# Scores at distances of 4 and 16 tokens: whole request rows in plain runs of columns instead of interleaved blocks with four columns in each skipped

## The chip, the cores and the metric

The kernel runs on one core of one Trainium2 chip, in one launch. The metric is the device time of the whole launch in microseconds (us); lower is better. Engines are named as in the profile: PE is TensorE (PEld its weight loads), DVE is VectorE, ACT is ScalarE, POOL is GpSimd, SP is SyncE, which here only issues DMAs.

## The reference

The program is a gated linear attention followed by two feed-forward layers:

```python
# q, k, v, alpha: batch 4, heads 8, sequence 768, head dim 48
for t in range(S):
    state = alpha[:, :, t, :, None] * state + einsum('bhd,bhe->bhde', k[:, :, t], v[:, :, t])
    y[:, :, t] = einsum('bhd,bhde->bhe', q[:, :, t], state)
x = y as (3072 tokens, 384)
h = x @ w_in;  x = (h * sigmoid(1.702 * h)) @ w_out       # 384 -> 2048 -> 384
h = x @ w_in2; out = (h - tanh(h)) @ w_out2               # 384 -> 2048 -> 384
```

All inputs and outputs are fp32.

## The kernel before

**Attention in chunks.** The sequence of a head is cut into 12 chunks of 64 tokens. Two batches with their eight heads (16 sequences, in 8 slots of two heads each) form a unit for one chunk; there are 24 units, each worked on as two items of half the slots, 48 items in all. Within a chunk the output of a token is a sum over earlier tokens of the same chunk, weighted by scores, and a part from the state of the chunk before. A score between two tokens needs the product of all alphas between them, so the kernel builds scores by levels: pairs that differ in the last base-4 digit of the token number (level 1), in the middle digit (level 4) and in the first digit (level 16). At each level the request rows (queries times alpha products) are made for digit distances 1, 2 and 3, and multiplied on PE with keys that carry the products on their side. The 64 tokens of a chunk lie in memory in the order `ORDER`, digits reversed.

**Request rows.** `R1`, `R4` and `R16` hold, for each slot, the columns for the three levels. Level 1 has plain runs of columns. `R4` has 112 columns a slot as four blocks of 28: 16 columns for distance 1, 8 for distance 2 and 4 for distance 3. `R16` has 112 columns as sixteen blocks of 7: 4, 2 and 1. A token whose digit is below the distance has no partner at it, so of the distance-1 columns of a block the first quarter is never used as a score. These columns exist all the same because the next products start from them. The views of these tiles are made in `views` (L368 to L388). The products are made by DVE for unit 0 in `first_unit` (L1082, product helper at L1087) and by POOL for the others in `first_part` and `second_part` (L519 and L548, product helper at L512). ACT copies the plain queries into the first 16 columns (L831).

**Scores on PE.** For an item PE runs `scores_1` (L618, 160 columns), the state products (L631), and then `scores_4_16` (L636): the matmuls at L645 take from `R4` the 24 used columns of each of the four blocks, those at L655 from `R16` the 6 used columns of each of the sixteen, so 96 moving columns in both. There are 8 matmuls of each line in an item, in two rounds of four. The four of a round go to four different quarters of the array (two halves of rows by two halves of columns, `TILES`). Each fp32 matmul shows in the trace as two instructions, so each line has 16 in an item and 768 in all. The results lie in PSUM as 96 columns for level 4 and 96 for level 16, block by block as in the request rows.

**Scores on DVE.** `scores` (L1034) builds the 64x64 score matrix of an item: one masked product for the diagonal (L1038), then nine predicated copies (L1056), three distances for each of the three levels, each with a mask of its own from the tile `MASK`. They are in a strict order (`put_step`); the fourth waits for `z_done`, which PE raises after `scores_4_16`. Destination, mask and PSUM source are all cut into blocks: 1 block at level 1, 4 at level 4, 16 at level 16.

**Order of the work.** The first two items (`LEAD`) are computed before any feed-forward product. All others are visits: `visits` (L128) gives each a place in the stream of feed-forward products on PE (L736, L741 up, L765 down; from the third token block on each fp32 product is three fp32r products). At a visit PE first finishes the item before (`item_outputs`: key transposes L604, state part L691, values L700), after waiting for its scores, then starts the next (`item_scores`). The stream is in program order, so all that PE does in a visit comes ahead of the next feed-forward product. The visits end near half of the span; after that PE runs feed-forward products only. Before the first feed-forward product SP sends the outputs of the first two items to HBM, loads them back as the first token block (`load_x`, L441), and behind that issues loads of alpha, queries, keys and the next weight groups (L317, L330) from one queue.

Of the kernel before, what the change touches and what calls it, by code (L numbers as in the profile page):

```python
# [37 lines left out]
PX = HS + D  # L38


def head_rows(hd):
    return slice(hd * HS, hd * HS + D)


C = 64
# [10 lines left out]
R1W = 64 + 32 + 16 + 64  # L56
S1W = R1W - 16
RW = 64 + 32 + 16
NW = 48 + 32 + 16
SLOT = 16  # L60

QP = 4
SL = 2 * QP
# [17 lines left out]
def level_masks():  # L81

    token = np.array(ORDER)
    j = np.tile(token, 2)[:, None]
    cols = []
    for h in (1, 4, 16):
        run = 4 * {1: 16, 4: 4, 16: 1}[h]
        for block in token.reshape(C // run, run):
            for dist in (1, 2, 3):
                cols.append(j // h == block[None, dist * run // 4:] // h - dist)  # L90
        if h == 1:
            cols.append(j == token[None, :])
    return np.concatenate(cols, axis=1).astype(np.int32)


MASK_AT = {1: 0, 4: S1W, 16: S1W + NW}
MASKW = S1W + 2 * NW


def item_of(j):  # L100
# [77 lines left out]
def build(nc, qT, kT, aT, vL, w_in1, w_out1, w_in2, w_out2, masks, ident, head, outT):  # L178
# [3 lines left out]
    with ctx:  # L182
# [27 lines left out]
        R4 = [sb(f"r4_{u}", [PX, SL, RW], where=att) for u in U2]  # L210
        R16 = [sb(f"r16_{u}", [PX, SL, RW], where=att) for u in U2]
# [12 lines left out]
        F4 = sb("f4", [PX, SL, 8, 4], where=att)  # L224
# [4 lines left out]
        MASK = sb("mask", [P, MASKW], I32, where=att)  # L229
# [7 lines left out]
        pZ = [pb(f"pZ{n}", [P, 4, 256]) for n in U2]  # L237
        pS1 = [x[:, :, 0:S1W] for x in pX]
        pP = [x[0:PX, :, S1W:S1W + D] for x in pX]
        pS4 = [z[:, :, 0:NW] for z in pZ]  # L240
        pS16 = [z[:, :, NW:2 * NW] for z in pZ]
        pY = [z[0:PX, :, 0:C] for z in pZ]
        pKT = [z[:, :, C:C + D] for z in pZ]
        pKT0 = [x[:, :, S1W + D:S1W + 2 * D] for x in pX]
# [5 lines left out]
        def buf(j):  # L250

            return int(j == 1)
# [30 lines left out]
        block = ctx.enter_context(nc.Block())  # L283
# [84 lines left out]
        def views(U):  # L368

            r1, r4, r16, q64 = R1[U % 2], R4[U % 2], R16[U % 2], Q64[U % 2]  # L370
            by4, by16 = (x[:].rearrange("p c (a x) -> p c a x", a=a) for x, a in ((r4, 4), (r16, 16)))
            r16 = r16[:]
            return Views(
                al=AL[:].rearrange("p (c s b) -> p c s b", c=SL, s=4),
                slot=r1[:, :, 0:7 * SLOT].rearrange("p c (k b) -> p c k b", b=SLOT),
                q=r1[:, :, R1W - C:R1W].rearrange("p c (s b) -> p c s b", s=4),
                qd4=by4[:, :, :, 0:16],
                v4=by4[:, :, :, 0:16],
                d4=by4[:, :, :, 16:24],
                e4=by4[:, :, :, 24:28],  # L380
                t4=T4[:].rearrange("p c s b -> p c (s b)"),
                pf4=F4[:, :, None, 0:4, :].to_broadcast([PX, SL, 4, 4, 4]),
                q16=r16.rearrange("p c (a b x) -> p c a b x", a=4, b=4)[:, :, :, :, 0:4],
                v16=by16[:, :, :, 0:4],
                d16=by16[:, :, :, 4:6],
                e16=by16[:, :, :, 6],
                pf16=F16[:, :, None, 0:4].to_broadcast([PX, SL, 16, 4]),
                q64=q64[:].rearrange("p (c a x) -> p c a x", c=SL, x=4))  # L388

# [120 lines left out]
        def _(pool):  # L510
            def mul(out, in0, in1):
                nc.gpsimd.tensor_tensor(out, in0, in1, ALU.mult).then_inc(q_step, 1)  # L512
# [35 lines left out]
            def second_part(U):  # L548
                base, tbase = U * Q_STEPS, U * T_STEPS
                r = views(U)  # L550
                pool.wait_ge(q_step, base + 5)
                pool.wait_ge(q4_copied, U + 1)
                pool.wait_ge(t_step, tbase + T_PF4)
                mul(r.q16, r.v4.rearrange("p c a (b x) -> p c a b x", b=4), r.pf4)
                mul(r.d4, r.v4[:, :, :, 8:16], r.t4[:, :, None, 4:12].to_broadcast([PX, SL, 4, 8]))
                pool.wait_ge(q_step, base + 6)
                pool.wait_ge(t_step, tbase + T_T16)
                mul(r.d16, r.v16[:, :, :, 2:4], T16[:, :, None, 1:3].to_broadcast([PX, SL, 16, 2]))
                pool.wait_ge(q_step, base + 7)
                mul(r.e4, r.d4[:, :, :, 4:8], r.t4[:, :, None, 4:8].to_broadcast([PX, SL, 4, 4]))  # L560
                pool.wait_ge(q_step, base + 8)
                mul(r.e16, r.d16[:, :, :, 1], T16[:, :, 1:2].to_broadcast([PX, SL, 16]))

                pool.wait_ge(t_step, tbase + T_SF16)
                if U >= 2:
                    pool.wait_ge(y_done, 2 * U - 2)
                nc.gpsimd.tensor_tensor(r.q64, r.v16, r.pf16, ALU.mult).then_inc(q64_ready, 1)
# [25 lines left out]
        def _(pe):  # L593
# [42 lines left out]
            def scores_4_16(j):  # L636
                U, pp = item_of(j)[:2]
                u = U % 2
                if pp == 0:
                    pe.wait_ge(q_step, U * Q_STEPS + Q_R4)  # L640
                    pe.wait_ge(k4_ready, U + 1)
                for q in range(2):
                    for h, z in TILES:
                        s = z * QP + 2 * pp + q
                        last = nc.tensor.matmul(pS4[buf(j)][z * C:(z + 1) * C, 2 * h + q, :].rearrange("p (a x) -> p a x", a=4),  # L645
                                                K4[u][head_rows(h), s * C:(s + 1) * C],
                                                R4[u][head_rows(h), s, :].rearrange("p (a x) -> p a x", a=4)[:, :, 4:],
                                                start=True, stop=True)
                if pp == 0:
                    pe.wait_ge(q_step, U * Q_STEPS + Q_R16)  # L650
                    pe.wait_ge(k16_ready, U + 1)
                for q in range(2):
                    for h, z in TILES:
                        s = z * QP + 2 * pp + q
                        last = nc.tensor.matmul(pS16[buf(j)][z * C:(z + 1) * C, 2 * h + q, :].rearrange("p (a x) -> p a x", a=16),  # L655
                                                K16[u][head_rows(h), s * C:(s + 1) * C],
                                                R16[u][head_rows(h), s, :].rearrange("p (a x) -> p a x", a=16)[:, :, 1:],
                                                start=True, stop=True)
                last.then_inc(z_done, 1)

            def item_scores(j):
# [278 lines left out]
        def _(dve):  # L940
# [93 lines left out]
            def scores(j, beside):  # L1034
                step = j * PUTS
                x = buf(j)
                dve.wait_ge(x_done, j + 1)
                nc.vector.tensor_tensor(AT[x], pS1[x][:, :, S1W - C:S1W],  # L1038
                                        MASK[:, None, S1W - C:S1W].to_broadcast([P, 4, C]), ALU.mult
                                        ).then_inc(put_step, 1)  # L1040
                puts = 0
                for h, ps in ((1, pS1[x]), (4, pS4[x]), (16, pS16[x])):
                    nb = C // (4 * {1: 16, 4: 4, 16: 1}[h])
                    run = C // nb
                    for dist in (1, 2, 3):
                        w = (4 - dist) * run // 4
                        at0 = (0, 3, 5)[dist - 1] * run // 4
                        dst = AT[x].rearrange("p k (b x) -> p k b x", b=nb)[:, :, :, dist * run // 4:run]
                        src = ps[:, :, 0:NW].rearrange("p k (b x) -> p k b x", b=nb)[:, :, :, at0:at0 + w]
                        msk = MASK[:, MASK_AT[h]:MASK_AT[h] + NW].rearrange("p (b x) -> p b x", b=nb)[:, :, at0:at0 + w]  # L1050
                        if h == 4 and dist == 1:
                            beside()
                            dve.wait_ge(z_done, j + 1)
                        puts += 1
                        dve.wait_ge(put_step, step + puts)
                        nc.vector.copy_predicated(dst, msk[:, None, :, :].to_broadcast([P, 4, nb, w]), src)\  # L1056
                            .then_inc(scores_ready if puts == PUTS else put_step, 1)
# [24 lines left out]
            def first_unit():  # L1082

                r = views(0)

                def mul(out, in0, in1):
                    nc.vector.tensor_tensor(out, in0, in1, ALU.mult).then_inc(q_step, 1)  # L1087
# [18 lines left out]
                dve.wait_ge(q_step, 5)  # L1106
                dve.wait_ge(q4_copied, 1)
                dve.wait_ge(t_step, T_T16)
                mul(r.q16, r.v4.rearrange("p c a (b x) -> p c a b x", b=4), r.pf4)
                mul(r.d4, r.v4[:, :, :, 8:16], r.t4[:, :, None, 4:12].to_broadcast([PX, SL, 4, 8]))  # L1110
                dve.wait_ge(q_step, 6)
                mul(r.d16, r.v16[:, :, :, 2:4], T16[:, :, None, 1:3].to_broadcast([PX, SL, 16, 2]))
# [103 lines left out]
```

## Time and profile before

| | |
|---|---|
| median of 3 runs | 978.55 us (978.42 to 978.98) |
| the profiled execution's own time | 978.98 us |
| its span, first to last instruction | 977.2 us |
| mean granted TensorE clock | 0.991 |
| PE busy | 952.2 us (97%) |
| DVE busy | 544.2 us (56%) |
| ACT busy | 334.1 us (34%) |
| POOL busy | 282.5 us (29%) |
| DMA | 59.07 MB, mean 60 GB/s |

The span is shorter than the execution's time by 1.8 us, which lie around the first and the last instruction. Busy time of an engine is time in which at least one of its instructions runs. The granted clock is a share of full speed: 1.00 stands for 2.4 GHz and 0.50 for 1.2 GHz. Durations of single matmuls overlap, since they are pipelined; what counts on PE is how far apart they start.

### The profile page before, as it was taken

The numbers are of one execution on the slowest core, as the hardware profiler recorded it, in microseconds if no ns is written. First come the engines' busy times: TensorE is split into PE (matmuls) and PEld (weight loads), VectorE is DVE, ScalarE is ACT, GpSimd is POOL, SyncE is SP. The second block draws the span as 40 slices with busy tenths as digits, with TensorE's granted clock in tenths as the row PEclk, the third lists the DMA queues.
The fourth block names the chain that finished last, engine by engine and source line by source line (L and its number), as shares of the span: only waits on it lengthen the run. The fifth ranks groups of instructions, "written<-read, shape, count | busy, mean of one in ns | idle before, by whom it ended". The sixth has DMA issues, their size and how long they took to land.

```text
span 977.2 us, 22232 instructions
## 1 busy us (share of the span) xinstructions
PE 952.2 (97%) x9342; PEld 823.7 (84%) x9342; DVE 544.2 (56%) x1349; ACT 334.1 (34%) x683; POOL 282.5 (29%) x314
## 2 busy tenths in 40 slices
PE   4799999999999999999999999999999999999998
PEld 3799999999999988888888888888888888888886
DVE  7679998878888877776321224334334333343333
ACT  2342333332332332323234554333333333333332
POOL 2554656555665655444001542000000000000000
PEclk9699999999999999999999999999999999999999
DMA  7833242332332432321113322020020010200000
GB/s 159 251 76 73 57 101 55 88 76 55 95 75 55 111 65 56 102 46 23 15 62 122 98 81 89 1 65 1 1 66 1 5 60 1 65 1 1 33 1 33
DMA packets 136533, 59.07 MB, mean 60 GB/s; under 512 B 114288, under 2 KB 131824, under 8 KB 136432
## 3 DMA queue, kind: packets, MB, share of 16 engines
q1 hardware_dynamic: 133616, 55.54, 22.6%
q10 hardware_dynamic: 2816, 2.10, 0.7%
q8 instruction: 74, 1.21, 0.5%
q14 instruction: 27, 0.22, 0.1%
HBM read 43.45 MB, written 14.16 MB: 59 GB/s over the span
## 4 chain that ended last, share of the span: by engine, by line
PE 94%; DVE 3%; DMA 1%; SPq 1%; issue 1%; ACT 0%; DVEq 0%; ACTq 0%
PE pX L741 38%; PE pZ L765 27%; PE pX L765 14%; PE pX L618 3%; PE pX L736 2%; PE pZ L700 2%; PE pZ L645 2%; PE pZ L604 2%; PE pZ L655 1%; PE pX L631 1%; PE pZ L691 1%; DVE scores L1056 1%; DMA w_raw<-w_out 1%; DVE w_lo L1062 1%; SPq L317 0%
## 5 line engine op out<-in xcount | busy, mean ns | idle before, releaser
L741 PE MATMUL pX<-x_hi,w_hi 128*128 128x512 f32 (+2 forms) x624 | 227.7, 365 | 0.7 <-ACT g L906 0.7
L741 PE MATMUL pX<-x_lo,w_hi 128*128 128x512 f32 (+2 forms) x624 | 227.3, 364 | 0.0
L741 PE MATMUL pX<-x_hi,w_lo 128*128 128x512 f32 (+2 forms) x624 | 227.3, 364 | 0.0
L1072 DVE TENSOR_TENSOR g_lo<-g,g_hi 128x512 fp32r<-128x512 f32 (+2 forms) x208 | 133.3, 641 | 155.0 <-ACT g_hi L911 154.8
L1171 DVE TENSOR_TENSOR g<-pX,sg 128x512 f32<-128x512 f32 x96 | 66.3, 691 | 177.7 <-ACT sg L908 177.7
L765 PE MATMUL pZ<-g_hi,w_hi 128*128 128x512 f32 (+2 forms) x414 | 151.0, 365 | 0.0
L765 PE MATMUL pZ<-g_lo,w_hi 128*128 128x512 f32 (+2 forms) x414 | 150.8, 364 | 0.0
L765 PE MATMUL pZ<-g_hi,w_lo 128*128 128x512 f32 (+2 forms) x414 | 150.8, 364 | 0.0
L911 ACT ACTIVATE g_hi<-g 128x512 fp32r<-128x512 f32 (+2 forms) x208 | 121.3, 583 | 78.0 <-DVE g L1171 74.5
L906 ACT ACTIVATE g<-pX 128x512 f32<-128x512 f32 (+3 forms) x144 | 65.6, 456 | 210.1 <-PE pX L741 175.9
L741 PEld LDWEIGHTS pX<-x_hi,w_hi 128*128 128x128 f32 x624 | 117.5, 188 | 17.8 <-ACT g L906 1.1
L741 PEld LDWEIGHTS pX<-x_lo,w_hi 128*128 128x128 f32 x624 | 117.5, 188 | 16.9
L741 PEld LDWEIGHTS pX<-x_hi,w_lo 128*128 128x128 f32 x624 | 117.5, 188 | 16.8
L908 ACT ACTIVATE sg<-pX 128x512 f32<-128x512 f32 x96 | 57.4, 598 | 181.9 <-PE pX L741 181.9
L512 POOL TENSOR_TENSOR r<-r,alpha 112x128 f32<-112x128 f32 (+2 forms) x115 | 109.2, 965 | 18.9 <-DMA r<-q_t 15.3
L1056 DVE COPY_PREDICATED scores<-mask,pZ 128x192 f32<-128x192 int32 (+2 forms) x282 | 105.7, 375 | 9.0
L765 PEld LDWEIGHTS pZ<-g_hi,w_hi 128*128 128x128 f32 x414 | 77.9, 188 | 11.3
L765 PEld LDWEIGHTS pZ<-g_lo,w_hi 128*128 128x128 f32 x414 | 78.0, 188 | 11.2
L765 PEld LDWEIGHTS pZ<-g_hi,w_lo 128*128 128x128 f32 x414 | 78.0, 188 | 11.2
L765 PE MATMUL pX<-g_hi,w_hi 128*128 128x512 f32 (+2 forms) x207 | 79.4, 384 | 0.0
L765 PE MATMUL pX<-g_hi,w_lo 128*128 128x512 f32 (+2 forms) x207 | 75.5, 364 | 0.0
L765 PE MATMUL pX<-g_lo,w_hi 128*128 128x512 f32 (+2 forms) x207 | 75.4, 364 | 0.0
(95 smaller groups left out, 1136.9 us busy)
## 6 DMA issues: line engine op xcount, KB each, us to landing
v<-v_l SPq DMA_DIRECT2D x96, 48.0 KB, 2.6
x_raw<-hidden SPq DMA_DIRECT2D x6, 768.0 KB, 5.8
attn_out<-y SPq DMA_DIRECT2D x94, 48.0 KB, 1.8
out_t<-o SPq DMA_DIRECT2D x10, 384.0 KB, 3.4
alpha<-a_t SPq DMA_DIRECT2D x24, 128.0 KB, 3.0
r<-q_t SPq DMA_DIRECT2D x24, 128.0 KB, 3.0
k<-k_t SPq DMA_DIRECT2D x24, 128.0 KB, 3.0
w_raw<-w_in SPq DMA_DIRECT2D x16, 192.0 KB, 2.4
```

The lines of the kernel that those rows point to most:

```text
L512: nc.gpsimd.tensor_tensor(out, in0, in1, ALU.mult).then_inc(q_step, 1)
L604: last = nc.tensor.matmul(out[z * C:(z + 1) * C, 2 * (h ^ z) + q, :], K64[U % 2][head_rows(h), s * C:(s + 1) * C], IDN[head_rows(h), :], s ...
L618: last = nc.tensor.matmul(pS1[buf(j)][z * C:(z + 1) * C, 2 * h + q, :], K1[u][head_rows(h), s * C:(s + 1) * C], R1[u][head_rows(h), s, SLO ...
L645: last = nc.tensor.matmul(pS4[buf(j)][z * C:(z + 1) * C, 2 * h + q, :].rearrange("p (a x) -> p a x", a=4), K4[u][head_rows(h), s * C:(s + ...
L741: last = nc.tensor.matmul(pH(N)[:, 0:w], win(wp, f, m), XS[T % 2][xp][:, m, 0:w], start=(n == 0), stop=(n == len(terms) - 1))
L765: last = nc.tensor.matmul(pO[m][:, 0:w], wt[:, m * P:(m + 1) * P], g, start=(f == 0 and n == 0), stop=(f == NF - 1 and n == len(terms) - 1))
L906: nc.scalar.activation(g_raw(N), H0[:, 0:width(T)], ACT.Gelu_apprx_sigmoid).then_inc(g_done, 1)
L908: nc.scalar.activation(SG[N % 2][:], pH(N), ACT.Tanh).then_inc(sg_done, 1)
L911: nc.scalar.activation(GH[:, columns(N)], g_raw(N), ACT.Copy).then_inc(gh_done, 1)
L1056: nc.vector.copy_predicated(dst, msk[:, None, :, :].to_broadcast([P, 4, nb, w]), src)\
L1072: nc.vector.tensor_tensor(GL[:, columns(N)], g_raw(N), GH[:, columns(N)].bitcast(F32), ALU.subtract).then_inc(gl_done, 1)
L1171: nc.vector.tensor_tensor(g_raw(N), pH(N), SG[N % 2][:], ALU.subtract).then_inc(g_done, 1)
```

## The change

The columns of `R4` and `R16` are laid out by distance: 64 columns for distance 1, 32 for distance 2, 16 for distance 3, each run in token order. Both matmuls read the whole 112 columns of a slot in one run and write 112 columns to PSUM, 16 of them (the distance-1 columns of tokens with digit 0) never read afterwards. The predicated copies of levels 4 and 16 skip these by a step (`skip`) at distance 1, and read mask and PSUM in a plain run at distances 2 and 3. Their destination, the number of elements and their count stay as they are. The masks grow by 2 x 16 columns. Level 1 is unchanged.

```diff
-NW = 48 + 32 + 16
@@ level_masks
+    digit = {1: np.arange(C) // 16, 4: np.arange(C) // 4 % 4, 16: np.arange(C) % 4}
     for h in (1, 4, 16):
-        run = 4 * {1: 16, 4: 4, 16: 1}[h]
-        for block in token.reshape(C // run, run):
-            for dist in (1, 2, 3):
-                cols.append(j // h == block[None, dist * run // 4:] // h - dist)
+        for dist in (1, 2, 3):
+            least = dist if h == 1 or dist > 1 else 0
+            i = token[digit[h] >= least][None, :]
+            cols.append(j // h == i // h - dist)
-MASK_AT = {1: 0, 4: S1W, 16: S1W + NW}
-MASKW = S1W + 2 * NW
+MASK_AT = {1: 0, 4: S1W, 16: S1W + RW}
+MASKW = S1W + 2 * RW
@@ PSUM views
-        pS4 = [z[:, :, 0:NW] for z in pZ]
-        pS16 = [z[:, :, NW:2 * NW] for z in pZ]
+        pS4 = [z[:, :, 0:RW] for z in pZ]
+        pS16 = [z[:, :, RW:2 * RW] for z in pZ]
@@ views
-                qd4=by4[:, :, :, 0:16],
-                v4=by4[:, :, :, 0:16],
-                d4=by4[:, :, :, 16:24],
-                e4=by4[:, :, :, 24:28],
+                qd4=r4[:, :, 0:C].rearrange("p c (s b) -> p c s b", s=4),
+                v4=r4[:, :, 0:C].rearrange("p c (a x) -> p c a x", a=4),
+                d4=r4[:, :, C:C + 32].rearrange("p c (a x) -> p c a x", a=4),
+                e4=r4[:, :, C + 32:RW].rearrange("p c (a x) -> p c a x", a=4),
-                q16=r16.rearrange("p c (a b x) -> p c a b x", a=4, b=4)[:, :, :, :, 0:4],
-                v16=by16[:, :, :, 0:4],
-                d16=by16[:, :, :, 4:6],
-                e16=by16[:, :, :, 6],
+                q16=r16[:, :, 0:C].rearrange("p c (a x) -> p c a x", a=4),
+                v16=r16[:, :, 0:C].rearrange("p c (a x) -> p c a x", x=4),
+                d16=r16[:, :, C:C + 32].rearrange("p c (a x) -> p c a x", x=2),
+                e16=r16[:, :, C + 32:RW],
@@ second_part (POOL) and first_unit (DVE)
-                mul(r.q16, r.v4.rearrange("p c a (b x) -> p c a b x", b=4), r.pf4)
+                mul(r.q16, r.v4, r.pf4)
@@ scores_4_16
-                        last = nc.tensor.matmul(pS4[buf(j)][z * C:(z + 1) * C, 2 * h + q, :].rearrange("p (a x) -> p a x", a=4),
+                        last = nc.tensor.matmul(pS4[buf(j)][z * C:(z + 1) * C, 2 * h + q, :],
-                                                R4[u][head_rows(h), s, :].rearrange("p (a x) -> p a x", a=4)[:, :, 4:],
-                                                start=True, stop=True)
+                                                R4[u][head_rows(h), s, :], start=True, stop=True)
...
-                                                R16[u][head_rows(h), s, :].rearrange("p (a x) -> p a x", a=16)[:, :, 1:],
-                                                start=True, stop=True)
+                                                R16[u][head_rows(h), s, :], start=True, stop=True)
@@ scores
-                        at0 = (0, 3, 5)[dist - 1] * run // 4
+                        if h == 1:
+                            at0, wide, skip = (0, 48, 80)[dist - 1], w, 0
+                        else:
+                            at0 = (0, C, C + 32)[dist - 1]
+                            wide, skip = (run, run // 4) if dist == 1 else (w, 0)
-                        src = ps[:, :, 0:NW].rearrange("p k (b x) -> p k b x", b=nb)[:, :, :, at0:at0 + w]
-                        msk = MASK[:, MASK_AT[h]:MASK_AT[h] + NW].rearrange("p (b x) -> p b x", b=nb)[:, :, at0:at0 + w]
+                        src = ps[:, :, at0:at0 + nb * wide].rearrange("p k (b x) -> p k b x", b=nb)[:, :, :, skip:wide]
+                        msk = MASK[:, MASK_AT[h] + at0:MASK_AT[h] + at0 + nb * wide]
+                        msk = msk.rearrange("p (b x) -> p b x", b=nb)[:, :, skip:wide]
```

## Rows read from the trace of the kernel before

**Rows 1.** The page: the chain that ended last, share of the span by engine.
```profile
PE 94%; DVE 3%; DMA 1%; SPq 1%; issue 1%; ACT 0%; DVEq 0%; ACTq 0%
```

**Rows 2.** Waits of PE: engine line <- releaser: us in total, times, longest us.
```profile
PE pX L736 <- ACT g L906: 5.0, 3, 4.2
...
PE pZ L604 <- DVE scores L1056: 0.6, 1, 0.6
```

**Rows 3.** PE by stretches: from:to length, busy (instructions), granted clock, DMA share, GB/s.
```profile
36.64:46.00 9.36, 8.63 (x119) 0.50 0.92 302
...
46.00:104.50 58.50, 58.50 (x1052) 1.00 0.39 87
104.50:114.00 9.50, 8.80 (x165) 1.00 0.23 43
114.00:353.00 239.00, 239.00 (x3920) 1.00 0.34 76
```

**Rows 4.** Single lines: instructions, duration ns min/median/max, first and last start, form.
```profile
L618 PE MATMUL pX<-r,k x768: 294/296/525, 7.9 to 472.7; 48*64 48x160 f32 x192
...
L691 PE MATMUL pZ<-q,state x704: 216/216/311, 42.7 to 482.3; 48*48 48x64 f32 x176
...
L645 PEld LDWEIGHTS pZ<-r,k x768: 129/133/228, 11.4 to 473.2; 48*64 48x64 f32 x192
L645 PE MATMUL pZ<-r,k x768: 242/243/419, 11.4 to 473.2; 48*64 48x96 f32 x192
...
L655 PE MATMUL pZ<-r,k x768: 242/242/365, 12.1 to 473.6; 48*64 48x96 f32 x192
```

**Rows 5.** The chain in one visit: start us, us that it advances, what.
```profile
60.69 0.23 PE pZ L691 x16
...
62.71 0.33 PE pZ L655 x16
```

**Rows 6.** The chain in the scores of the first two items, same columns.
```profile
13.10 0.38 DVE scores L1056
...
16.85 0.38 DVE o L1056
...
17.26 0.31 DVE o L1056
...
17.59 0.24 DVE o L1056
...
17.85 0.45 DVE o L1056
...
18.32 0.45 DVE o L1056
...
18.80 0.44 DVE o L1056
```

**Rows 7.** Timeline around first score products: start, us, engine, line, out<-in, count.
```profile
11.09 0.28 DVE L1087 TENSOR_TENSOR r<-r,t 112x128 f32<-112x128 f32 x1
...
11.29 0.38 DVE L1087 TENSOR_TENSOR r<-r,t 112x128 f32<-112x128 f32 x1
...
12.12 0.86 PE L655 MATMUL pZ<-r,k 48*64 48x96 f32 x16
```

**Rows 8.** The chain behind the first two items, same columns.
```profile
23.51 0.41 SPq L317
...
28.18 7.69 DMA w_raw<-w_out
```

**Rows 9.** The chain from 99 us to 114 us, start us, us, what.
```profile
100.73 0.34 DVE scores L1038
...
109.89 0.35 DVE scores L1038
...
113.96 0.45 PE pZ L604 x16
```

**Rows 10.** Waits of POOL, as in group 2.
```profile
POOL k L527 <- DVE g_lo L1072: 100.3, 18, 7.8
```

More of the change, by code:

```diff
@@ L370, in views @@
             r1, r4, r16, q64 = R1[U % 2], R4[U % 2], R16[U % 2], Q64[U % 2]
-            by4, by16 = (x[:].rearrange("p c (a x) -> p c a x", a=a) for x, a in ((r4, 4), (r16, 16)))
-            r16 = r16[:]
             return Views(
@@ L376, in views @@
                 q=r1[:, :, R1W - C:R1W].rearrange("p c (s b) -> p c s b", s=4),
-                qd4=by4[:, :, :, 0:16],
-                v4=by4[:, :, :, 0:16],
-                d4=by4[:, :, :, 16:24],
-                e4=by4[:, :, :, 24:28],
+                qd4=r4[:, :, 0:C].rearrange("p c (s b) -> p c s b", s=4),
+                v4=r4[:, :, 0:C].rearrange("p c (a x) -> p c a x", a=4),
+                d4=r4[:, :, C:C + 32].rearrange("p c (a x) -> p c a x", a=4),
+                e4=r4[:, :, C + 32:RW].rearrange("p c (a x) -> p c a x", a=4),
                 t4=T4[:].rearrange("p c s b -> p c (s b)"),
-                pf4=F4[:, :, None, 0:4, :].to_broadcast([PX, SL, 4, 4, 4]),
-                q16=r16.rearrange("p c (a b x) -> p c a b x", a=4, b=4)[:, :, :, :, 0:4],
-                v16=by16[:, :, :, 0:4],
-                d16=by16[:, :, :, 4:6],
-                e16=by16[:, :, :, 6],
+                pf4=F4[:, :, 0:4, :].rearrange("p c s b -> p c (s b)")[:, :, None, :].to_broadcast([PX, SL, 4, 16]),
+                q16=r16[:, :, 0:C].rearrange("p c (a x) -> p c a x", a=4),
+                v16=r16[:, :, 0:C].rearrange("p c (a x) -> p c a x", x=4),
+                d16=r16[:, :, C:C + 32].rearrange("p c (a x) -> p c a x", x=2),
+                e16=r16[:, :, C + 32:RW],
                 pf16=F16[:, :, None, 0:4].to_broadcast([PX, SL, 16, 4]),
@@ L654, in scores_4_16 @@
                         s = z * QP + 2 * pp + q
-                        last = nc.tensor.matmul(pS16[buf(j)][z * C:(z + 1) * C, 2 * h + q, :].rearrange("p (a x) -> p a x", a=16),
+                        last = nc.tensor.matmul(pS16[buf(j)][z * C:(z + 1) * C, 2 * h + q, :],
                                                 K16[u][head_rows(h), s * C:(s + 1) * C],
-                                                R16[u][head_rows(h), s, :].rearrange("p (a x) -> p a x", a=16)[:, :, 1:],
-                                                start=True, stop=True)
+                                                R16[u][head_rows(h), s, :], start=True, stop=True)
                 last.then_inc(z_done, 1)
@@ L1108, in first_unit @@
                 dve.wait_ge(t_step, T_T16)
-                mul(r.q16, r.v4.rearrange("p c a (b x) -> p c a b x", b=4), r.pf4)
+                mul(r.q16, r.v4, r.pf4)
                 mul(r.d4, r.v4[:, :, :, 8:16], r.t4[:, :, None, 4:12].to_broadcast([PX, SL, 4, 8]))
```

## The prediction

> **What bounds the kernel now.** I read the page's busy times and chain first. PE is busy for 97% of the span (the table above) and makes up 94% of the chain that ended last, against 3% for DVE [rows 1]. So I read the PE side in two views: who PE waits for, and how full it is by stretches. From 46.0 to 104.5 us and from 114 to 353 us PE has no idle time [rows 3]. Between them lie 0.70 idle us [rows 3], of which 0.6 are one wait for a DVE score copy [rows 2], ahead of the visit at 113.96. Ahead of 46 us the order of things is another one: the chain runs through DVE's work for the first two items [rows 6], then through SP's queue and a weight load that lands 7.69 us after its issue [rows 8], and PE waits 4.2 us for what comes of it [rows 2]. The reader is to see three regimes: a head that DVE's products and copies set, a weight load whose start they set, and from about 36 us a PE stream in which every added nanosecond of PE counts.
>
> **Part 1, wider matmuls (adds, on the path).** L645 and L655 go from 96 to 112 moving columns. A column's price: the 160-column instruction takes 296 ns, the 96-column one 243 [rows 4], 53 ns for 64 columns, 0.83 ns a column, so 13.2 ns for 16. The four quarters of the array work beside each other, so the price is paid once for four instructions, four times for the 16 of a line. The chain agrees: L655 advances it by 0.33 us for its 16, L691 with 64 columns by 0.23 [rows 5], 0.10 us for 32 columns, 0.05 for 16. I take 4 x 13.2 = 53 ns a line, 0.106 us a visit. PE's program order puts it ahead of the next feed-forward product, and nothing of PE's idle time hides it.
> Of 48 items, items 0 and 1 lie in the head, and item 2 (at 29 us) ends before the 4.2 us wait, so it costs nothing. Item 3 runs at about 45 us at granted clock 0.50, the 1.2 GHz level [rows 3], where a column costs double: 0.2 us. The other 44 run at 1.00: 44 x 0.106 = 4.65 us. Sum +4.85 us.
> The unknown is whether the old reads in pieces (24 of 28, or 6 of 7 columns) cost something that a plain run doesn't. Two lines with plain runs stand on both sides: L691 with 64 columns takes 216 ns, L618 with 160 takes 296 [rows 4]. The straight line between them gives 242.7 ns at 96 columns, and L645 and L655 have 243 and 242. So the pieces cost nothing, whether of 24 or of 6, and 112 columns will take 256. Ends: the chain's 0.10 us is read to 0.01, so 0.045 to 0.058 us a line, or +4.1 to +5.3 in the sum; for a gain the pieces would have to cost what the straight line excludes (rival B).
>
> **Part 2, DVE's predicated copies (less time).** In item 1 the three copies of level 4 took 0.38, 0.31 and 0.24 us, for 192, 128 and 64 elements a partition. Those of level 16, with the same numbers of elements, took 0.45, 0.45 and 0.44 [rows 6]. The time of level 16 doesn't follow the elements: it has 64 pieces of 3, 2 and 1. After the change mask and source are plain runs at distances 2 and 3, and the destination stays in pieces. From both sides: nothing if the destination sets the price; 0.07 + 0.14 + 0.20 = 0.41 us an item if all three fall to level 4's times. The nearest row for one side of it: the product of 128 elements that is written and read in steps of 7 took 0.38 us, the one in pieces of four 0.28 [rows 7], 0.8 ns an element. So I put distance 2 at 0.33 and distance 3 at 0.27 and leave distance 1 at 0.45, where all three streams keep their pieces. That is 0.29, I take 0.3 us an item. Level 4 stays: its pieces cost nothing now.
> The Trainium skill (SBUF — State Buffer, section "Door 1: The DMA port swizzle", the note on cachelines) says that SBUF is read in lines of 16 bytes and PSUM in lines of 8, and that each step to a new line costs. The trace agrees in kind for DVE, as far as 0.44 against 0.24 us for 64 elements shows it. By it the stepping destination would keep a price, which lies between my ends.
> Where does the saving count? In the steady stretch DVE has half its time free, so nowhere, but for two places.
> *Head.* The chain runs through both items' copies. The product in steps of 7 (L1087 at 11.29) gives back 0.1 us, but the fourth copy of item 0 starts at 13.10, and PE's L655 ends at 12.12 + 0.86 = 12.98 [rows 6, 7]. So the fourth copy waits for PE already. PE there is slower: L655 takes 0.86 us from start to end; less 0.36 for the last instruction (the longest of its line, 365 ns [rows 4]) that is 0.50 for three rounds, against 0.25 in the warm visit. Double price for both lines is +0.2 us, so item 0's fourth copy comes 0.2 us later, and the 0.1 us is lost. Head: +0.2 - 2 x 0.3 = -0.4 us (ends +0.2 and -0.6). What follows (the outputs' way to HBM, `load_x`, the queue of SP and the weight load [rows 8]) all starts from there and moves as a whole.
> *The wait near 113.4.* The chain is on DVE without a break from 96 us on, through the scores of two items, at 100.73 and 109.89 [rows 9]. They give back 0.6 us, and PE comes 0.1 us later for one visit in between. The 0.7 idle us vanish: -0.7 us (ends -0.1 and -0.7). What is late next is PE itself.
>
> **Part 3, POOL and ACT, the same number of products.** Units 1 to 23 have their products on POOL. It waits 100.3 us for DVE's `g_lo` as its signal to start [rows 10], and no wait of PE names POOL. Their price can rise or fall with the new pieces; up to tenths of a us a unit the cover is this free time, and I put it at nothing. Should the cover be gone, PE's L645 would wait for `R4` at a visit. ACT's copy keeps its shape. The masks' load grows by 16 KB and lies beside the head's other loads. No wait and no DMA is added.
>
> **Sum.** +4.85 - 0.4 - 0.7 = +3.75 us on the profiled execution's own 978.98 us (977.2 in its span and 1.8 around it): 982.7. That execution was the slowest of three, 0.43 above the median; for a median I take 982.3.
>
> **Rivals.**
> *A: DVE gives back nothing,* since the destination in pieces sets the copies' time. For it: all three streams step today, so no row tells them apart. Against: the row with 0.8 ns an element. Then head +0.2, the wait near 113.4 loses only 0.1: +4.85 + 0.2 - 0.1 = +4.95, 983.5.
> *B: reads in pieces cost PE something, and the plain run is quicker although longer* (faster than before). Place: the 16 instructions of L655 in each visit. As a mechanism: if each piece cost two columns' time to begin, L655 with sixteen pieces would take the time of 128 columns today and L645 with four that of 104. On plain runs of 112 the one would fall by 0.053 us and the other grow by 0.027, so 0.026 less a visit, 1.2 us less for 44, and 1.1 less from DVE: 976.2. In all it decides from 1.1 ns a piece: 44 x 4 x 20 pieces x 1.1 ns are the 3.75 us of my sum. By the note of the Trainium skill named above pieces that cross its lines cost. The trace doesn't show it on PE. Against: the straight line through the plain rows, and the equal 242 and 243 ns.
> *C: the added columns are hidden,* because a round of four is set by its weight loads. For it: a weight load takes 133 ns [rows 4], longer than a round. Against: a round of L691 takes 0.23 / 4 = 0.058 us and one of L655 0.33 / 4 = 0.083 [rows 5], so the columns set it. Then only DVE's part is left: 978.55 - 1.1 = 977.5.
> *D: the stretch at clock 0.50 changes.* It lasts from 36.64 to 46.00 here, after PE's 4.2 us of waiting [rows 3, 2]. The head shifts this by tenths of a us. If it is shorter or longer by a third, 3 us, half of that is won or lost: 982.3 -+ 1.5, 980.8 or 983.8. For it: the granted clock is 0.50 there and 1.00 behind it. Against: three runs within 0.56 us.
>
> **Chances and range.** Forecast 0.70 (its own range 981.6 to 983.0), A 0.14, D 0.09 (half each way), B 0.03, C 0.04. The range of 980.9 to 984.2 holds the forecast, A and nearly all of D. About 0.2% (1.96 us) is what a measurement can tell from no change: slower begins at 980.5. The forecast, A and D lie above it, with 0.02 off for errors in them: slower 0.91. C lies within, with 0.02 more for a forecast that comes out too high: same 0.05. Faster 0.04 is B and a remainder.
>
> **What would show it.** In the profile after: L645 and L655 with 112 columns and 256 ns in the median, and an advance of 0.38 us for 16 in the chain; busy time of PE up by about 5 us; L1056's copies at level 16 at 0.45, 0.33 and 0.27 in the head; no PE wait for `scores` near 114; the weight load issued about 0.4 us earlier than 28.18. It is wrong if L645 stays at 243 ns, if the last visit isn't 3 to 4 us later than now, or if a new wait of PE on POOL appears.

## The result, and the profile after

The changed kernel takes 983.84 us in the median of 4 runs (983.41 to 984.12), the kernel before 978.48 beside it (977.23 to 978.98). The ratio is 1.0055, with a 95% interval of 1.0041 to 1.0070. A second group gave 983.13 against 979.33, ratio 1.0039 (1.0027 to 1.0052). The change makes the kernel slower, by 5.4 us in the first group and by 3.8 in the second. Forecast was 982.3, with 981.6 to 983.0 for the mechanism that was forecast and 980.9 to 984.2 in all: the median lies in the whole range and above the forecast's own.

The profiled execution after took 982.78 us with a span of 981.0, 3.8 us more than before. The last visit's L645 began at 473.2 us, its L643 now begins at 476.8, and PE is busy for 958.0 us against 952.2. The two PE lines are now L643 and L652. First their durations, as in [rows 4], then the chain in the visit that answers to [rows 5], with L645 of the kernel before in a fence of its own.

```profile
L643 PE MATMUL pZ<-r,k x768: 256/256/446, 11.1 to 476.8; 48*64 48x112 f32 x192
...
L652 PE MATMUL pZ<-r,k x768: 256/256/391, 11.9 to 477.2; 48*64 48x112 f32 x192
```

```profile
60.33 0.23 PE pZ L687 x16
...
61.91 0.49 PE pZ L643 x16
62.40 0.38 PE pZ L652 x16
```

```profile
62.27 0.44 PE pZ L645 x16
```

256 ns against 242 and 243, and 0.49 us against 0.44 and 0.38 against 0.33 for the 16 of a line, are what was forecast: 0.05 us a line. From the first start of L645 (L643) to the next feed-forward product it is 821 ns in the median of the visits before and 928 after, 0.107 us a visit.

The level-16 copies of item 1 in the chain of waits, as in [rows 6] (distances 1, 2 and 3; ahead of them the fourth copy of item 0, behind PE):

```profile
11.12 1.03 PE pZ L643 x16
12.14 0.79 PE pZ L652 x16
...
12.96 0.38 DVE scores L1057
...
17.72 0.46 DVE o L1057
...
18.20 0.45 DVE o L1057
...
18.67 0.45 DVE o L1057
```

The copies are not as forecast. Mask and source are plain runs at distances 2 and 3 now, and the copies take as long as before: 0.45 us each. In the head nothing is given back, and the wider matmuls cost there what was forecast: item 0's fourth copy, which waited for PE before the change too, starts 7.13 us after the first product (5.83 to 12.96) where it was 6.97 (6.13 to 13.10).

PE by stretches, as in [rows 3], and its wait for the scores:

```profile
36.82:44.40 7.58, 6.85 (x75) 0.50 0.78 238
44.40:46.00 1.60, 1.60 (x64) 0.99 1.06 382
46.00:104.50 58.50, 58.50 (x1033) 1.00 0.38 88
104.50:114.00 9.50, 9.31 (x183) 1.00 0.24 43
114.00:353.00 239.00, 239.00 (x3862) 1.00 0.34 76
```

```profile
PE pZ L602 <- DVE scores L1057: 0.2, 1, 0.2
```

From 104.5 to 114 us 0.19 us are idle, where it was 0.70. And in this execution the granted clock was 0.99 from 44.4 us on, where the kernel before had 0.50 until 46.0: the work of 1.6 us at 1.2 GHz takes 0.8 us at 2.4 GHz, so this execution won 0.8 us by it.

The way from the first product to the first feed-forward product behind the weight load, in the kernel before and in that after (the weight load before is in [rows 8]):

```profile
6.13 0.69 DVE r L1087
...
36.64 1.66 PE pX L736 x6
```

```profile
5.83 0.69 DVE r L1088
...
27.98 8.07 DMA w_raw<-w_out
...
36.82 1.66 PE pX L732 x6
```

The visit behind that stretch, in the chain of the kernel before and in that after:

```profile
52.03 0.38 PE pZ L604 x16
```

```profile
51.56 0.38 PE pZ L602 x16
```

The sum of the spans: -0.5 up to this visit, of which -0.8 are the clock level and +0.3 all else. Of these 0.3, 0.18 stand at that feed-forward product (36.82 against 36.64): the queries' load landed 0.3 us earlier, the head's products and scores took 0.18 longer, the weight load was issued 0.20 earlier all told but took 8.07 us in place of 7.69. The rest is the added columns of item 3. From here it is +4.7 for 44 visits and -0.5 for the wait. That is 3.7 of the 3.8. The profiled 982.78 is below all other runs of this kernel (983.22 to 984.12). The 0.8 us of the clock may be the reason, but the other runs have no stretches to compare, so it is not shown.

### The profile page after: what moved, and what is told of

The parts are those of the page before. It is cut to its first block, busy times and chain, and to the rows that moved or that the text cites. A ratio compares the mean times of both kernels' runs of the same rounds, so it can differ in the third digit from the quotient of the medians.

```text
span 981.0 us, 22232 instructions
## 1 busy us (share of the span) xinstructions
PE 958.0 (98%) x9342; PEld 827.8 (84%) x9342; DVE 533.7 (54%) x1349; ACT 334.1 (34%) x683; POOL 279.2 (28%) x314
## 4 chain that ended last, share of the span: by engine, by line
PE 94%; DVE 3%; DMA 1%; SPq 1%; issue 0%; ACT 0%; ACTq 0%; DVEq 0%
PE pX L737 38%; PE pZ L761 27%; PE pX L761 14%; PE pX L616 3%; PE pZ L643 2%; PE pZ L696 2%; PE pX L732 2%; PE pZ L652 2%; PE pZ L602 2%; PE pX L629 1%; PE pZ L687 1%; DVE scores L1057 1%; DMA w_raw<-w_out 1%; DVE w_lo L1063 1%; SPq L317 0%
## 5 line engine op out<-in xcount | busy, mean ns | idle before, releaser
L1073 DVE TENSOR_TENSOR g_lo<-g,g_hi 128x512 fp32r<-128x512 f32 (+2 forms) x208 | 135.7, 652 | 159.9 <-ACT g_hi L907 159.7
```

The source lines that it names most:

```text
L1073: nc.vector.tensor_tensor(GL[:, columns(N)], g_raw(N), GH[:, columns(N)].bitcast(F32), ALU.subtract).then_inc(gl_done, 1)
```

## The experiments

**The changed kernel again,** as the base of the group.

> The changed kernel itself, beside the others of this group. Theory P (the 16 added columns of both PE lines are the whole loss; 44 visits of 0.107 us, DVE's copies give back nothing since their destination sets their time): 983.0 to 984.0 us, +0.45 to +0.6% against the kernel before, copies of level 16 at 0.45 us each. Rival Q (part of the loss lies elsewhere, in the new layout's effect on the head's products and copies): the same time, so this run only gives the base for the others.

Measured 983.13 us (5 runs, 981.43 to 983.94) against 979.33 (16 runs), 1.0039 (1.0027 to 1.0052). The time is at the low end of the expected range; the ratio is below the expected +0.45 to +0.6%.

**The PE part taken back, the layout left.** 96 of the 112 columns in one plain run:

```diff
-    matmul(pS4[...][..., 2 * h + q, :], K4[...], R4[u][head_rows(h), s, :])
+    matmul(pS4[...][..., 2 * h + q, 0:96], K4[...], R4[u][head_rows(h), s, 0:96])
     ... the same for level 16
-    at0 = (0, C, C + 32)[dist - 1]
+    at0 = (0, C, C + 16)[dist - 1]
```

> The changed kernel with both PE lines cut to the first 96 of the 112 columns of a slot, in one plain run; the distance-3 copies take columns of distance 2 instead, so the distance-3 scores are not computed. Everything on DVE and POOL keeps shape and count. Theory P: PE's price goes back to 83 ns a round of four, a visit to 2.73 us, and the time to that of the kernel before, 978.5 us (within 0.1%). Rival Q: what the layout does outside PE stays, so 979.5 to 980.5. Rival B of the prediction (pieces cost PE something): a plain run of 96 is quicker than the pieces of 96 of the kernel before, a round below 80 ns and a time below 977.

Measured 978.16 us (11 runs), ratio to the kernel before 0.9992 (0.9983 to 1.0001). Its L652 and the visit:

```profile
L652 PE MATMUL pZ<-r,k x768: 242/243/365, 11.7 to 473.0; 48*64 48x96 f32 x192
```

```profile
61.87 0.44 PE pZ L643 x16
62.31 0.33 PE pZ L652 x16
```

The distance-3 scores are left out, with all shapes on DVE kept. The loss is gone with the 16 columns. A plain run of 96 takes the same 242 to 243 ns and 0.33 us as the pieces of 6 before, so rival B has nothing here. What the layout alone is worth is between -0.17% and +0.01%: not told from nothing.

**The PE part alone.** The kernel before, with the whole blocks multiplied:

```diff
-    R4[u][head_rows(h), s, :].rearrange("p (a x) -> p a x", a=4)[:, :, 4:]
+    R4[u][head_rows(h), s, :]
     ... the same for R16; PSUM ranges of 112 columns
-    src = ps[:, :, 0:NW].rearrange(...)[:, :, :, at0:at0 + w]
+    cols, over = (NW, 0) if h == 1 else (RW, run // 4)
+    src = ps[:, :, 0:cols].rearrange(...)[:, :, :, over + at0:over + at0 + w]
```

> The kernel before with only the PE part of the change: both lines read all 112 columns of a slot and write them to PSUM block by block; the copies skip the first quarter of each block; masks, layout of R4 and R16 and all products as before. Theory P: a round of 96 ns, a visit of 2.84 us and the time of the changed kernel, 983.8 us (+0.5%). Rival Q: less than the changed kernel by what its layout costs, 982 to 983.

Measured 983.39 us (5 runs), 1.0047 (1.0033 to 1.0060), beside 1.0039 of the changed kernel. The time is 0.4 us below the 983.8 of theory P and not below that of the changed kernel, as rival Q had it. The wider matmuls alone bring the whole loss. With the run before, this is an edit done alone and an edit undone, and they agree.

**Columns taken away further,** down to 80:

```diff
+    ... 2 * h + q, 0:80], ... R4[u][head_rows(h), s, 0:80]; the same for level 16
-    at0 = (0, C, C + 32)[dist - 1]
+    at0 = (0, C - 16, C)[dist - 1]
```

> The changed kernel with both PE lines cut to the first 80 of the 112 columns of a slot (distance 2 and 3 copies take columns that are there, so their scores are wrong; the count and shapes of all else stay). Theory P (0.83 ns a column, in every visit): a round of 70 ns, a visit 0.21 us shorter than with 112, 44 visits 9.4 us, 0.3 more in the head and the cold visit, and 0.1 to 0.2 back as a longer DVE wait near 113: 973.5 to 974.5, -0.5%. Rival C of the prediction (weight loads set a floor for a round): the round stays above 75 ns and the time above 976.

Measured 975.05 us (6 runs) against 978.62, 0.9960 (0.9946 to 0.9974). The time came out 0.5 us above the expected range; the price of a column did not:

```profile
L652 PE MATMUL pZ<-r,k x768: 229/229/338, 11.9 to 468.7; 48*64 48x80 f32 x192
```

```profile
61.75 0.28 PE pZ L652 x16
```

80, 96 and 112 columns: 229, 242 and 256 ns; 0.28, 0.33 and 0.38 us a line. The price is a straight line, and weight loads of 133 ns set no floor down to 80, so rival C is out. Most of the missing half microsecond is waiting: PE comes earlier and DVE does not, and PE is idle for 0.13 us between 100 and 104 us and for 0.63 between 112 and 114, 0.76 where the changed kernel has 0.19 and 0.1 to 0.2 more had been counted on. The rest stays open.

**The copies' destination made plain in the changed kernel:**

```diff
     dst = AT[x].rearrange("p k (b x) -> p k b x", b=nb)[:, :, :, dist * run // 4:run]
+    if h == 16:
+        dst = AT[x][:, :, 0:nb * w].rearrange("p k (b x) -> p k b x", b=nb)
```

> The changed kernel with the three level-16 copies written to one plain run of 48, 32 and 16 columns of the score matrix (the wrong places, so the level-16 scores are misplaced); sources and masks untouched. Theory P: the destination alone sets their time, so 0.37, 0.30 and 0.23 us instead of 0.45 each; the head gets 2 x 0.4 us shorter and the wait near 113.5 us goes, 983.8 - 0.8 - 0.2 = 982.8. Rival R (the pieces of source and mask share in the price): distance 2 and 3 stay over 0.4 us here as they did when only source and mask became plain, and the time stays at 983.8.

Measured 981.85 us (6 runs), 1.0030 (1.0018 to 1.0041); that is 1.3 us below the changed kernel beside it, where 1.0 was expected. The level-16 copies of item 1 in its chain:

```profile
17.48 0.38 DVE o L1059
...
17.88 0.31 DVE o L1059
...
18.21 0.23 DVE o L1059
```

The destination alone had held them at 0.45. PE has no wait for scores near 113 any more. From the first product to the end of item 1's scores the head takes 12.50 us (5.94 to 18.44) in place of 13.29.

**The same edit in the kernel before,** whose masks and sources are in pieces:

> The kernel before, where source and mask of the level-16 copies are in pieces, with the destination made one plain run of 48, 32 and 16 columns (the level-16 scores are misplaced). The last corner of a square whose others are measured: all in pieces 0.45, only the destination in pieces 0.45, only distance 1's source in pieces 0.38. Theory P (the destination alone counts): 0.38, 0.30 and 0.23 us although all sources and masks are in pieces; the head gets 2 x 0.4 us shorter and the 0.6 us wait near 113 goes: 979.3 - 1.4 = 977.9. Rival R (pieces anywhere keep the price): 0.45 us each and 979.3.

Measured 978.23 us (12 runs) against 978.62, 0.9992 (0.9982 to 1.0002): 0.4 us, not told from nothing, where 1.4 were expected. Its copies:

```profile
17.28 0.39 DVE o L1058
...
17.69 0.35 DVE o L1058
...
18.07 0.27 DVE o L1058
```

The four corners for distances 2 and 3: 0.45 and 0.44 us with all in pieces, 0.45 and 0.45 with only the destination in pieces, 0.35 and 0.27 with only mask and source in pieces, 0.31 and 0.23 with nothing in pieces. The prices do not add up. The dearest stream sets the time and hides the other. So the change took away the cheaper of two costs that lay beside each other. Theory P is right as long as the destination is in pieces; once it is plain, the pieces of mask and source, which were not parted, show with 0.04 us.

And the 0.6 us wait near 113 did not go, although DVE saved 0.3 us an item. A timeline of that stretch of this run (start, us, engine, line; in brackets the idle time before and what ended it):

```profile
93.43 7.44 POOL L512 TENSOR_TENSOR r<-r,alpha 112x256 f32<-112x256 f32 x1
...
100.94 1.26 SPq L317 DMA_DIRECT2D alpha<-a_t  x2
...
104.74 0.94 DVE L952 TENSOR_TENSOR sf<-alpha 112x128 f32<-112x128 f32 x1 [0.25 <-DMA alpha<-a_t]
```

```profile
PE pZ L604 <- DVE scores L1058: 0.6, 1, 0.6
```

DVE came early, found the alphas of the next unit not yet loaded (SP issues the load when POOL has read the old ones, and POOL's product had ended at 100.87), waited 0.25 us and then took 0.94 us for a product that the kernel before did in 0.28 at this place. The saving was spent there.

The five products of POOL that end with this one, in the kernel before and in this run:

```profile
90.30 3.73 POOL L512 TENSOR_TENSOR r<-r,alpha 112x512 f32<-112x512 f32 x5
```

```profile
90.44 10.43 POOL L512 TENSOR_TENSOR r<-r,alpha 112x512 f32<-112x512 f32 x5
```

When POOL's last one ran long can be read from the eleven profiled executions of all versions. It goes with how its start lies to that of DVE's product of keys (L1001, in the changed kernel L997). In eight of them POOL begins 0.15 to 0.22 us before DVE (93.29 and 93.49 us in the kernel before); then POOL's takes 0.73 us and DVE's 1.06 to 1.13. In three they begin within 0.05 us of each other (93.43 and 93.44 in this run; the other two are the changed kernel with the plain destination and the run in steps of 2 and 4 columns below); then DVE's takes 0.69 us and POOL's 7.38 to 7.48. Here DVE had come nearer to POOL by 0.19 us than in the kernel before, which is less than one item's saving.

In the head DVE saved 0.6 us (12.49 from the first product to the end of item 1's scores, against 13.11), and the weight load was issued at 27.11 us in place of 28.18. But it took 8.56 us, and the first feed-forward product behind it came 0.20 us earlier (36.44). Over the eleven profiled executions this load took 7.14 to 8.56 us, and an earlier issue did not mean an earlier landing: issued at 27.11 in this run it landed at 35.67, issued at 27.50 in the second group's run of the changed kernel at 34.64. So no trace shows that tenths won in the head reach the feed-forward products.

**Pieces of one column on PE.** The kernel before, level 16 read in another order:

```diff
-    out ... .rearrange("p (a x) -> p a x", a=16)
-    R16 ... .rearrange("p (a x) -> p a x", a=16)[:, :, 1:]
+    out ... .rearrange("p (x a) -> p x a", a=16)
+    R16 ... .rearrange("p (a x) -> p x a", a=16)[:, 1:, :]
```

> The kernel before with level 16's 96 moving columns read in another order: six groups of 16 single columns that lie 7 columns apart, where it was sixteen pieces of 6 (so level-16 scores come out in the wrong order). Same count of columns. Theory P: PE reads pieces of any length at the same pace: a round stays at 83 ns, the visit at 2.73 us, the time at 979.3. Rival B in its general form (each piece costs PE something): 96 pieces in place of 16; at 1 ns each a round grows by 80 ns, a visit by 0.3 us, the time by 14 us.

Measured 994.11 us (4 runs) against 978.62, 1.0157 (1.0140 to 1.0174): 15.5 us more, where rival B in its general form had 14.

```profile
61.92 0.44 PE pZ L645 x16
62.36 0.70 PE pZ L655 x15
```

Theory P's sentence that PE reads pieces of any length at the same pace is wrong. The same 96 columns take 0.70 us for 15 of 16 instructions where pieces of 6 take 0.33. Rival B's fixed price for each piece is no rule either, since the pieces of 6 cost nothing. My forecast of "the pieces cost nothing" was right for the pieces of this kernel, and not as a rule. Two more orders follow, with one run each beside one of the kernel before (978.34 us); there the lines of the trace are what is read. In all three the result goes to PSUM in one plain run, so the order of reading is what changed.

**Steps of 2 and 4 columns** in the changed kernel (`"p (a x) -> p x a"` on source and result, `x=2` for level 4 and `x=4` for level 16):

> The changed kernel, all 112 columns, read by PE in another order: level 4 in single columns 2 apart (8 bytes), level 16 in single columns 4 apart (16 bytes); the scores of both levels come out in the wrong order. Looked at is the length of a round of four in the trace. The run with single columns 7 apart (28 bytes) took 176 ns for 96 columns, where pieces of 6 took 83. Theory S (what counts is that a piece has one column): both lines 200 ns or so. Theory L (what counts is the distance in bytes, and up to 16 bytes it is free): both 96 ns, as in plain order. Theory H (each column pays by how many lines of memory it opens): 96 ns for 2 apart and 200 for 4 apart.

Measured 1002.90 us (one run).

```profile
63.77 0.51 PE pZ L643 x16
64.28 0.80 PE pZ L652 x16
```

112 columns 2 apart take 0.51 us against 0.49 in plain order; 4 apart they take 0.80 against 0.38. Of the three theories only H has both.

**Pieces of two and three columns** in the kernel before (`"p (a x y) -> p x a y"`, `y=2` for level 4, pieces 28 columns apart; `y=3` for level 16, 7 apart):

> The kernel before, 96 columns, with other pieces: level 4 in pieces of two columns that begin 28 columns apart, level 16 in pieces of three that begin 7 columns apart; the scores of both levels come out in the wrong order. Theory S (only single columns pay): both rounds 83 ns. Theory H (a piece pays a fixed time to open its memory line, about 1.8 ns in an instruction of single columns, hidden if the columns of the piece take as long, 0.83 ns each): pieces of two just over the edge, 88 to 95 ns, pieces of three 83. Theory B (each piece costs 1.1 ns, hidden by nothing): 48 pieces 136 ns, 32 pieces 118 ns.

Measured 981.65 us (one run).

```profile
61.99 0.46 PE pZ L645 x16
62.44 0.39 PE pZ L655 x16
```

Pieces of two: 0.46 against 0.44. Pieces of three: 0.39 against 0.33, where theory H had no price and theory B had 0.47. H holds for singles and twos. For the threes it needs an addition: 7 apart, some of them straddle a boundary of 4 columns (16 bytes) and some do not. As an estimate: counting each 16-byte stretch that a piece touches (1.5 for a piece on average, 48 in all) at the 0.80 / (4 x 112) us = 1.8 ns of the steps of 4 gives 86 ns a round, 0.35 us a line. Measured is 0.39, so the count explains a part, and the rest stays open. For pieces of 6 it gives 36 stretches, 65 ns, hidden under the 80 ns that 96 columns take at 0.83 ns each.

## Why the prediction was right or wrong

**Part 1, the columns: right, in size too.** 0.053 us a line, 0.106 a visit, 44 visits; measured 0.05 and 0.107, and the runs with the PE part alone and without it carry the whole loss. The line through the plain rows of 64 and 160 columns gave 256 ns for 112, which is what they take.

**Part 2, the copies: wrong.** The step that failed is "So I put distance 2 at 0.33 and distance 3 at 0.27". They stayed at 0.45, so the 0.3 us an item that DVE was to give back were nothing. I took the price of a destination in steps from a product (L1087, 0.8 ns an element) although that is another instruction that reads and writes SBUF; the predicated copy takes 0.45 us for a destination in 64 pieces, and hides its sources beside that. The end of the range that I had put against it, nothing given back, was what happened. That makes -0.4 us in the head into +0.2: from the first product to the end of item 1's scores the kernel before takes from 6.13 to 19.24 us, 13.11, the changed one from 5.83 to 19.12, 13.29. The head's PE term (+0.2, since the fourth copy already waited for L655) was right, also in that it swallowed the 0.1 us of the product at L1087. That the head then "moves as a whole" is not shown: the weight load's own time differs by more than the head's terms.

**The wait near 113.4: right in sign, for another reason, and too large.** I had it vanish by 0.7 us because DVE would be faster. It fell by 0.5 in the profiled execution although DVE's copies were not faster. Two things made it shorter. DVE's last copy ended at 113.65 us in place of 113.92; its way there from the first of the two items took as long as before (13.12 us from 100.53, against 13.19 from 100.73), but began 0.20 us earlier, in an execution whose PE had won 0.8 us by the clock. The rest is PE, which comes later by its added columns, as it does in the kernel before with only the PE part of the change, where the wait is 0.4 us. That a faster DVE alone need not shorten it is seen in the kernel before with a plain destination: the time went into a wait for the alphas.

**Part 3, POOL and ACT: right.** POOL's busy time is 279.2 us against 282.5, ACT's 334.1 in both, and no wait of PE names POOL.

**The rivals.** A is what came true, with 983.5 us against 983.84; it had 0.14. B is a true mechanism of this chip at pieces of one and, in part, three columns, but it costs nothing at pieces of 6 and 24, as its counter-argument said. C is out by the straight line from 80 to 112 columns. D came true in part in the profiled execution, where the clock came back at 44.4 us in place of 46.0, worth 0.8 us. In the eleven profiled executions of all versions it came back between 43.6 and 46.6 us, early and late ones with either layout; whether the change shifts it is not told by so few. The chances had a slip of their own: C's 0.04 with 0.02 more are 0.06 for "same", not 0.05.

The sum with the measured terms in place of mine is +4.85 + 0.2 - 0.5 = +4.6 us. The two groups measured +5.4 and +3.8. That the profiled execution, with 982.78 us, met the 982.7 forecast for it is luck: the missing savings, some 0.8 us in head and wait, were made up by the 0.8 us of the clock.

No version here that computes all scores beats the kernel before. The one with 80 columns takes less time (0.9960) and leaves scores out; 96 plain columns with the new layout are at 0.9992 (0.9983 to 1.0001) and leave out the scores of distance 3.

## What to carry to other kernels

Streaming a few unused columns to get a plain access pattern is a trade of time on the matmul engine for simplicity, and where that engine is the bound each column has its price whatever the pattern was; look first whether the pieces cost anything, by a line through rows with plain patterns. When an instruction has several streams in pieces, making some of them plain gives nothing as long as the dearest one stays, so find the dearest by changing one stream at a time. A saving on an engine that runs in step with loads has to be followed to the next thing it waits for, and to what it now runs beside, before it is counted.

## What the runs showed of the hardware that I had not expected

PE reads a moving fp32 operand at full pace (0.83 ns a column for a round of four) only as long as consecutive columns lie close. In steps of 8 bytes it takes 0.51 us for a line of 112 against 0.49, in steps of 16 bytes 0.80 us against 0.38, 1.8 ns a column; in steps of 28 bytes 0.70 us for 15 of 16 instructions with 96 columns, 1.8 ns again. The Trainium skill (SBUF — State Buffer, section "Door 1: The DMA port swizzle", the note on cachelines) has 16-byte lines that want at least two hits each. The trace agrees: two hits a line are nearly free, one is not. It also speaks of strides of up to four fp32 as free; for a step of four on PE the measurement is 0.80 against 0.38 us and decides.

A predicated copy on DVE takes 0.45 us for 64 destination pieces, whether they hold 3, 2 or 1 elements, and 0.23 to 0.38 us for the same elements in a plain destination; 16 pieces cost nothing.

One POOL product of 256 elements a partition lasted 7.44 us in the run shown above, where the mean of its form is 1.37 us in that run and 0.86 us in the kernel before. DVE ran its products and `w_lo` differences back to back in that time. In the kernel before it is the DVE product that waits: 1.08 us in place of 0.69, beside a POOL product of 0.73 that began 0.20 us ahead of it. Spans on POOL are rough in a trace; SP's issue at 100.94, which waited for this product, bears the end out. The load of alphas that waited for its end landed at 104.74, late for DVE.
